# A mixture-of-experts tail: one copy, one weight load and one row load moved

## The reference

```python
x = attention(q, k, v)                  # 4 x 8 heads, 576 positions, block-causal mask
x = softplus(x @ moe_w_in) @ moe_w_out  # 2304 rows, 512 -> 2048 -> 512
skip_score = x @ w_skip
do_compute = skip_score > 0
out = x.copy()
xc = x[do_compute]
logits = xc @ w_gate
e_idx = np.argmax(logits, axis=1)       # one of 8 experts
gate_w = softmax(logits)[chosen]
for e in range(8):                      # h = relu(xc @ w1[e]); y = gate_w * (h @ w2[e])
    ...
out[do_compute] = xc + y
```

## Time and profile before

| | us |
|---|---|
| median of 3 runs (727.57 to 729.45) | 728.22 |
| the profiled execution | 723.76 |
| its span, first to last instruction | 721.9 |
| TensorE busy | 685.2 (95%) |
| VectorE busy | 430.4 (60%) |
| ScalarE busy | 404.6 (56%) |
| GpSimd busy | 161.4 (22%) |
| mean granted TensorE clock | 0.983 of 2.4 GHz |

### The profile page before, as it was taken

One profiled execution on the slowest core, in us unless ns is written; L12 is line 12 of the kernel. 1 busy time (PEld: TensorE's weight loads), 2 busy tenths in 40 slices (PEclk: granted clock), 3 DMA queues, 4 the chain that ended last, 5 costly groups with the idle time before them and its releaser, 6 DMA issues.

```text
span 721.9 us, 13187 instructions
## 1 busy us (share of the span) xinstructions
PE 685.2 (95%) x4114; PEld 533.8 (74%) x4114; DVE 430.4 (60%) x1048; ACT 404.6 (56%) x990; POOL 161.4 (22%) x224
## 2 busy tenths in 40 slices
PE   7999999999979999999999999999999999988684
PEld 5565656565569989889988888899888988744352
DVE  5676767676546576577657765776677667533011
ACT  3676666666656566556665665656556655412121
POOL 2867676767710000010002000200020001011011
PEclk8999999999999999999999999999999999989898
DMA  9455755553120000100200020002000100594400
GB/s 205 103 155 136 198 140 146 145 149 111 50 85 1 2 0 35 55 8 3 69 19 8 1 87 0 0 0 87 0 12 0 44 0 3 188 380 137 177 24 17
DMA packets 79537, 53.76 MB, mean 74 GB/s; under 512 B 61192, under 2 KB 64264, under 8 KB 79488
## 3 DMA queue, kind: packets, MB, share of 16 engines
q1 hardware_dynamic: 76032, 50.73, 23.6%
q0 software_dynamic: 1776, 1.33, 0.7%
q10 hardware_dynamic: 1680, 1.08, 0.6%
HBM read 41.18 MB, written 16.28 MB: 80 GB/s over the span
## 4 chain that ended last, share of the span: by engine, by line
PE 62%; DVE 4%; issue 3%; ACTq 1%; ACT 1%; DVEq 0%; POOL 0%; POOLq 0%
PE hidden L931 9%; PE rows_out L944 9%; PE hidden L933 9%; PE rows_out L942 9%; PE hidden L932 9%; PE rows_out L943 8%; PE rows_out L1054 3%; PE hidden L1037 3%; PE turned_y L969 1%; DVE log L1327 1%; PE rows_out L1046 1%; DVE g L1328 1%; PE misc L978 1%; DVE series L1324 1%; PE misc L987 0%
## 5 line engine op out<-in xcount | busy, mean ns | idle before, releaser
L931 PE MATMUL hidden<-x_parts,w_in_high 128*128 (+1 forms) x384 | 132.6, 345 | 2.4 <-DVEq L1330 2.2
L1154 ACT ACTIVATE mag<-hidden 128x384 f32<-128x384 f32 x96 | 47.1, 491 | 151.1 <-PE hidden L933 150.9
L933 PE MATMUL hidden<-x_parts,w_in_low 128*128 (+1 forms) x384 | 129.5, 337 | 0.0
L932 PE MATMUL hidden<-x_parts,w_in_high 128*128 (+1 forms) x384 | 129.4, 337 | 0.0
L944 PE MATMUL rows_out<-w_out_high,g_low 128*128 128x512 f32 x288 | 114.1, 396 | 0.0
L942 PE MATMUL rows_out<-w_out_high,g_high 128*128 128x512 f32 x288 | 113.7, 395 | 0.4 <-DVE g_low L1337 0.4
L883 POOL DMA_INDIRECT x_sorted<-y,slot x18 | 20.4, 1132 | 418.3 <-DVE slot L1379 414.7
L943 PE MATMUL rows_out<-w_out_low,g_high 128*128 128x512 f32 x288 | 113.5, 394 | 0.0
L931 PEld LDWEIGHTS hidden<-x_parts,w_in_high 128*128 128x128 f32 x384 | 72.2, 188 | 10.7 <-DVEq L1330 3.5
L444 ACT ACTIVATE probs<-scores,neg_max 128x128 f32<-128x128 f32 (+3 forms) x128 | 67.0, 529 | 21.6 <-DVE neg_max L520 17.8
L266 POOL TENSOR_SCALAR probs<-probs,inverse 128x128 f32<-128x128 f32 (+3 forms) x128 | 65.6, 532 | 52.6 <-DVE inverse L541 52.6
(11 more groups left out here) (174 smaller groups left out, 1073.8 us busy)
## 6 DMA issues: line engine op xcount, KB each, us to landing
whole_w<-in_moe_w_dram SPq DMA_DIRECT2D x12, 1024.0 KB, 11.2
x_heads<-x_pair SPq DMA_DIRECT2D x16, 288.0 KB, 2.1
x_raw<-x_heads SPq DMA_DIRECT2D x6, 768.0 KB, 5.7
out_dram<-y SPq DMA_DIRECT2D x6, 768.0 KB, 4.0
q_nat<-in_q_dram SPq DMA_DIRECT2D x32, 128.0 KB, 2.8
v_nat<-in_v_dram SPq DMA_DIRECT2D x32, 128.0 KB, 2.4
stage<-in_moe_w_in_dram SPq DMA_DIRECT2D x8, 512.0 KB, 3.8
stage<-in_moe_w_out_dram SPq DMA_DIRECT2D x8, 512.0 KB, 3.7
```

What stands on the lines that cost most here:

```text
L931: nc.tensor.matmul(o, win["high"][:, k, cols], high, start=(k == 0), stop=False)
L932: nc.tensor.matmul(o, win["high"][:, k, cols], low, start=False, stop=False)
L933: last = nc.tensor.matmul(o, win["low"][:, k, cols], high, start=False, stop=(k == K - 1))
```

## The change

Three moves. The copy of the third early tile's rows on VectorE goes from in front of `choose` and `place` to behind the second signal of `tally_ready`. On SyncE a wait is added before the late weights: when there were early tiles and place 0 has tiles left, SyncE waits until TensorE has finished the first half of the hidden product of the first later tile. On ScalarE `load_ahead` goes from the middle of a later tile to its end. No product, no transfer and no buffer is added or taken away.

```diff
@@ -837,6 +837,11 @@
             sp.wait_ge(s["hidden_ready"], F * BLOCKS)
             sp.wait_ge(s["g_used"], F * BLOCKS)
             early_tiles = all_early(sp)
+
+            with sp.If(early_tiles > 0):
+                with sp.If(entry(sp, TILES_LEFT, 0) > 0):
+                    sp.wait_ge(c["hidden_ready"], 2 * early_tiles + 1)
+                    sp.sem_inc(c["waited"], 1)
             for p in range(E):
                 with sp.If(entry(sp, LOAD, p) > 0):
                     if p >= SLOTS:
@@ -1293,10 +1298,10 @@
                     tile = early_tiles + number
                     relu(tile, 0)
                     copy_hT(tile, 0)
-                    load_ahead(number, tile)
                     relu(tile, 1)
                     copy_hT(tile, 1)
                     copy_xT(turns + number + 1)
+                    load_ahead(number, tile)
             act.wait_ge(c["later_x_loaded"], 16 * (later_tiles + AHEAD))
             act.sem_inc(c["waited"], 1)
 
@@ -1530,14 +1535,14 @@
             early_tiles = all_early(dve)
             with dve.If(early_tiles > 0):
                 copy_x(1, early_row(1))
-                with dve.If(early_tiles > 2):
-                    copy_x(2, early_row(2))
             choose(BLOCKS - 1)
             place(BLOCKS - 1)
             dve.wait_ge(s["slots_ready"], BLOCKS)
             step.then(nc.vector.tensor_copy(tiles[:, FIRST_FREE:FIRST_FREE + E], base[0:1, 0, :]))
             dve.sem_inc(s["tally_ready"], 1)
             with dve.If(early_tiles > 0):
+                with dve.If(early_tiles > 2):
+                    copy_x(2, early_row(2))
                 finish(0, early_row(0))
             later_tables()
             with dve.If(early_tiles > 2):
```

## The result

| | before | changed |
|---|---|---|
| median, us (4 runs each) | 728.75 (727.57 to 729.45) | 719.88 (718.38 to 720.92) |
| the profiled execution | 723.76 | 718.96 |
| its span | 721.9 | 717.1 |

The ratio of the medians is 0.9878, 95% interval 0.9852 to 0.9904: 8.9 us faster. The forecast was 719.7. But the two profiled executions differ by 4.8 us only, where the sum had 8.5 between them. The median was met, and the sum was not; what follows is mostly about that. The size of the gain does not hold everywhere either: in a later set of runs, on another occasion, the same two kernels differ by 3.3 us (720.63 and 717.30, ratio 0.9952, interval 0.9929 to 0.9975).

What follows compares the result with a forecast made beforehand. TensorE was taken to bound the kernel, busy 95% of the span, with idle waits in the last 95 us. 2.8 + 3.9 + 3.0 - 1.2 = 8.5 us off 723.76 gave 715.3; plus 4.5, 719.7 (8-in-10 range 716.8 to 724.6).

Steps and rivals of the forecast that it cites:

- three signs of being wrong: Far branch still 4 us or more; a tile 4 turn waiting for a row load; half clock beyond the one stretch.
- Part 1, 2.8 us: Early tiles: moving VectorE's copy lets TensorE turn the later rows near 659.75 instead of 662.60, 2.8 us gained.
- two limits agree: Turn of later rows: TensorE's own chain arrives at 659.7, as does the chain through closing stores and row loads.
- all of this moves by 1.45: Closing stores and later row loads come 1.45 us earlier, so VectorE's copy of the rows ends at 659.6.
- Part 2, 3.9 us: Gap between the series: without late weights moving, TensorE's far branch falls from 6.26 to 2.32 us, 3.9 gained.
- the branch stays long: Rival in the gap between the series: the read is slow anyway, 3.9 us less gain, 723.6 us; 10%.
- The burst's new company: Late weights beside tiles 3 to 5 with a row load and a store: cost taken as 0, bounds 0 to 4.8 us.
- second rival: Burst holds the first row load or a store; TensorE waits 4.8 us at the turn, 724.5 us; 14%.
- The clock, 1.2 us lost: Behind the shorter gap the half-clock stretch covers more work: 1.2 us lost, bounds minus 1.35 and plus 2.0.
- The rival of a second stretch: Second half-clock stretch in tiles 1 to 2 from the 0.8 and 1.6 us gaps: up to 3.3 us, 723.0; 10%.
- Part 3, 3.0 us: Later tiles: row load at tile's end removes four TensorE waits for the relu, 3.0 us gained, bounds 2.4 to 3.4.
- Nothing in the sum touches the difference: The median's 4.5 us above the profiled execution was assumed to remain, turning 715.3 into a forecast of 719.7.

Runs made afterwards that it cites:

- third set: Later runs on another chip, with the changed kernel unchanged, part 1 alone and a six-product filler beside the kernel before, which took 720.63 us.
- without_copy: Parts 2 and 3 without part 1, against the kernel before: 718.72 us, ratio 0.9946.
- only_copy_again: Part 1 alone (VectorE's copy moved) once more, against the kernel before on another chip: 719.86 us, ratio 0.998.
- the burst: Changed kernel plus four unneeded 1 MB loads where the late weights were issued before, against the kernel before: 721.05 us, ratio 0.9992.
- after_again: The changed kernel, unedited, run again on another chip against the kernel before: 717.30 us, ratio 0.9952.
- first set: Runs of the kernel before, unchanged, and of each part alone, on one chip; the kernel before takes 728.7 us; the main result is counted with it.
- before_again: The kernel before, unchanged, profiled again and timed against itself: 728.48 us, ratio 0.9998.
- only_weights: Part 2 alone (late weights behind the first later hidden product), against the kernel before: 724.76 us, ratio 0.9941.
- only_rows: Part 3 alone (ScalarE loads rows at a tile's end), against the kernel before: 724.89 us, ratio 0.994.
- after: The changed kernel with all three parts, against the kernel before: median 719.88 us, profiled execution 718.96 us.
- without_weights: Parts 1 and 3 without part 2, against the kernel before: 719.90 us, ratio 0.9972.

## Why the prediction was right, and where it was not

The forecast of the median was met to 0.2 us, by two errors that cancel. The paths that it named are the right ones; the sizes of parts 1 and 2, and the step from the profile to the median, are not. Of the three signs of being wrong that it gave, two came: a turn in tile 4 waited for a row load (0.17 us), and the clock stood at 0.50 in a second stretch. The third, a branch of 4 us or more, did not.

- **Part 1, 2.8 us: the path was right, the size depends on the execution.** Ranks without a wait at 640.03, an idle time of 0.41 for 0.8 before tile 1 and of 1.87 for 1.6 in it: close to the forecast. (The prediction's "657.8" for the turn that TensorE could reach does not follow from its own 5.4 us, which give 657.2; only with that do its two limits agree.) The step "all of this moves by 1.45" failed in the profiled execution: SyncE began the closing stores 1.8 us earlier and needed 1.8 us more for the six (9.52 for 7.69), so the row loads left at 656.60 for 656.50, and of the 2.85 us only 1.28 came, of which 0.44 is common. In the third set the turn came 2.5 us earlier, the common part taken off. A gives the same: the gain is 2.5 us against a kernel before with the half-clock stretch in tile 1 (34.0 to 31.5) and 1.4 against without_copy, which has none (32.9 to 31.5). The medians of the third set leave it between nothing and 3.0 us (only_copy_again).
- **Part 2, 3.9 us: right mechanism, one term mis-sized.** The branch "near 2.3" measured 3.39, and where no bulk load was in flight 3.29 to 3.33 in five further traces and 3.8 in two: the two far branches at the end, of 2.2 to 2.9 us, are not the same jump and were the wrong rows to price it by. At the end the read starts with the branch (within 0.1 us of it in 25 of 28, at most 0.6 behind it); between the series it starts 0.93 us behind it, in those two traces 1.4 to 1.5. From the start of the read to the end of the branch it is 2.3 to 2.8 us at both places. So what the sum lacked is the time ahead of the read, some 0.9 us; what fills it is open. Worth 2.9 us, not 3.9, and the gap is 6.11 and 5.77 us, not 4.8. The rival "the branch stays long" is out by part 2 alone, by the kernel without it, and by the burst.
- **The burst's new company: close to the point from which it costs.** The row load took 6.0 us to land, as the store of the earlier trace rows had it, and 6.8 and 7.0 us in two further traces; the turn in tile 4 waits 0.17, 1.02 and 1.25 us. The prediction gave 6.7 us as the point, and took 0. These three pairs put the point near 5.8 us, and the cost is 0.2 to 1.25 us, a small form of the second rival. The weights left at 677.16, not 673.5: tile 3 began at 669.74, where "6.5 to 7 us earlier" meant 666.7 to 667.2, and the 16 products that they wait for ran at 1.2 GHz and ended near 673.4; the 3.8 us behind them are as forecast. They were all there by 692.4, 7.7 us before the last tile.
- **The clock, 1.2 us lost: met in this trace.** The 24 hidden products took 5.39 us for 4.11, 1.3 us more, and the turn behind them another 0.1. But in after_again they took 4.18, with a stretch of 3.4 us in place of 6.8: the clock after the gap differs between executions. The rival of a second stretch came (648.2 to 651.6), yet cost nothing in the end, because TensorE waits for the rows at 661.32 anyway.
- **Part 3, 3.0 us: right.** The four waits of 0.96, 0.87, 0.59 and 0.59 us are gone in every kernel with it, and B falls by 3.1 us with it alone.
- **The tail, which the sum left alone**, is 8.3 us for 7.6; its two far branches took 2.57 and 2.71 us for 2.32 and 2.28. The code of the tail is the same in all these traces, and it is 7.6 to 8.6 us long in them.
- **Sum for the profiled execution:** 1.3 (with the common 0.4) + 2.6 (gap) + 3.0 - 1.4 (clock) - 0.2 (tile 4) - 0.7 (tail) = 4.6 of the 4.8 seen; 8.5 were forecast.
- **From the profile to the median.** "Nothing in the sum touches the difference" was the step that should have failed and was saved by chance. The 4.5 us between the profiled execution of before and its median are, by the one usual execution that was profiled, a stall in tiles 1 and 2. The changed kernel does not have it in full: its median is 0.9 above its profile. The shortfall of the sum (3.7) and this (3.6 less) cancel. That was luck. In the third set, where no trace has the stall, the change is worth 3.3 us (1.8 to 5.1), and there a forecast of minus 8.5 would have been wrong by 5.

What stays open: what makes the first set's kernels stall. In all its traces but that of before, SyncE is slow in the closing stores (9.1 to 9.5 us for 7.7), and the records of the single stores show one hole, of 2.6 to 3.9 us, between the second and the third. In before_again, only_weights and only_rows ScalarE stops at about the same time: the relu of tile 1 starts 3.5 to 4.3 us after its product, and 3.7 to 3.8 us after ScalarE's own stores. In only_rows SyncE's hole is from 648.0 to 651.9 and ScalarE's from 648.3 to 652.1. I have no experiment that turned it on or off, and the chip itself is a rival that no run rules out. Also open is how much of the 13.1 us that the parts have by themselves in that set is this stall moving about.

## What to carry to other kernels

A far branch waits for a read of instructions, and bulk loads in flight hold the start of that read (by some 3 us here): keep them out of the microseconds before a loop change, and start them on a signal that the next loop is under way. Before a profiled execution is used as the base of a forecast, compare it with the median of the runs: where it is 4 us off, those are 4 us of something that the change may touch. Repeat the comparison in another set before the size of a gain is believed: this one was 8.9 us in one and 3.3 in another. And a gap ahead of a tile can cost twice, once as idle time and again as work at 1.2 GHz behind it. The gap between the series (5.8 us and more) did so in the 12 traces that have it whole; a wait of 2.39 us before the ranks did in some traces and not in without_copy. Three spare products in the gap took the second cost away in the one execution that was profiled with them.

## What the runs showed of the hardware

- A far branch with its 16 KB read took 2.2 to 2.9 us at the kernel's end, 3.3 to 3.8 between the series, and 6.2 to 6.7 with 4 MB of loads in flight. The difference is nearly all ahead of the read: it starts with the branch at the end (at most 0.6 us behind it), 0.9 to 1.5 us behind it between the series, and 3.7 to 4.2 us behind it in that company. From its start to the end of the branch it was 2.3 to 2.8 us in every case.
- How long TensorE ran at 1.2 GHz behind the gap between the series differed between executions with nearly the same gap: 6.8 us in after, behind a gap of 6.11, and 3.4 in after_again, behind one of 5.77.
- Issuing the same six closing stores took SyncE 7.5 to 7.7 us in nine traces and 9.1 to 9.5 in five, all of the first set, with the longer time in one hole behind the second store.
- A row load of 128 KB beside the late weights landed after 6.0 to 7.0 us. Issued in the middle of a tile with no weights moving it landed after 2.5 to 2.7 us (before, before_again, only_copy_again), at a tile's end after 2.5 to 3.6 (without_weights).
